# When transposed probabilities are filled and multiplied with V in an attention and mixture-of-experts kernel

## The chip, the cores and the metric

The kernel runs on one core of one Trainium2 chip. The metric is the device time of one execution in microseconds (us), lower is better. Besides plain runs there is one execution under the hardware profiler, whose records the profile and the trace show.

## The reference, cut to what matters

```python
def _attn_ref(q, k, v, f):                      # 4 batches, 8 heads, S = 576, D = 64
    scores = np.matmul(q, k.transpose(0, 1, 3, 2)) / np.sqrt(D)
    cum = np.cumsum(np.log(np.clip(f, 0.0001, 1.0)), axis=-1)
    scores = np.where(causal, -1e9, scores + cum[..., :, None] - cum[..., None, :])
    attn = np.exp(scores - np.max(scores, axis=-1, keepdims=True))
    attn = attn / (np.sum(attn, axis=-1, keepdims=True) + 1e-09)
    return np.matmul(attn, v)
```

Its output, 2304 tokens of 512 numbers, goes through a dense feed-forward layer (512 to 2048 and back, with a piecewise quadratic in between) and then through a layer of eight experts of which each token takes one. The change touches the attention and the first steps of the feed-forward part.

## The kernel before, in words

The attention works on 16 pairs of heads, and each pair on 9 tiles of 64 queries (both heads side by side, so 128 rows). There are 144 steps, n = 9 * pair + tile, and each engine has its own loop over n, written out by hand; semaphores alone join them. Every multiplication is done in three passes of a high and a low part, to keep float32 accuracy.

Tile i of a pair passes through these stages:

- PE scores it (`score`, L1304 to L1314, causal, so 64 * (i + 1) columns, and a small matmul that adds the mask) four steps ahead, n + 4. Tile 8 is too wide for one bank and has six matmuls of 288 columns (L1310).
- DVE adds the decay and takes the row minimum (`masked`, L984), three steps ahead.
- ACT takes the exponential (`exp`, L783), two steps ahead.
- PE transposes the probabilities in blocks of 128 x 128 into one of two PSUM banks (`turn`, L1329). One call is a *fill*; there are eight in a pair, numbered 0 to 7, with 2, 4, 4, 2, 4, 4, 4 and 1 transpositions, and fill k takes bank k % 2. A fill waits until DVE has emptied the bank from the fill two before (`pt_l`). Fills 0 to 7 need tiles up to 1, 3, 5, 5, 7, 7, 8 and 8.
- ACT copies a fill as the high part (`high`, L792), and DVE subtracts to get the low part (`low`, L1000), which frees the bank.
- PE multiplies with V: an early product for tiles 0 to 3 of both heads (`attend_early`), and for tiles 4 to 8 the late product a of one head and b of the other (`attend_late_a`, `attend_late_b`), all at L1345. ACT copies the early product (L798), DVE the two late ones (L1012, L1016).

Behind the last fill PE transposes the inverse denominators of the pair before (`turn_inverse`, L1337; *inverse* in short), and DVE copies them (L1006). DVE computes the denominator with its 1e-9 at tile 7 (L990) and inverts at tile 8 (L996).

Which fill runs in which step comes from the table `FILL`, whose first field is the tile that the fill needs last:

```python
FILL = ((1, 0, 1, 0, 2), (3, 0, 2, 2, 2), (5, 0, 2, 4, 2), (5, 2, 1, 4, 2),
        (7, 0, 2, 6, 2), (7, 2, 2, 6, 2), (8, 0, 4, 8, 1), (8, 4, 1, 8, 1))
```

So before, fill 0 is at tile 1, fill 1 at 3, fills 2 and 3 at 5, fills 4 and 5 at 7, fills 6 and 7 at 8, and none at tiles 0, 2, 4 and 6. The early product stands at tile 6, the late products of the pair before at tiles 2 and 4.

POOL splits q, k and v of the coming pairs into high and low parts: kh (L566), qh (L568), kl (L570), ql (L573), then v (`split_v`, L581 and L583). `split_v` waits for `late_b` of two pairs before, as it overwrites V. In eight pairs (6 to 13) one block of the attention's output is read back, multiplied on POOL with the inverse denominators (L622, L624), and split by ACT (L804) and DVE (L1021, the x split) at tile 1 of the next pair; the next such load waits for the DVE split. SP issues the loads and stores.

At the end, PE has two up blocks of the feed-forward part (12 matmuls each) at steps 142 and 143, and the DVE's first `hidden` stand at steps 146 and 148. A `hidden` is a chain of DVE hclip (L1026), ACT hpos and hsq (L829, L831), DVE g (L1029), ACT gh (L839) and DVE gl (L1031); PE needs hpos to take the up block's bank again.

## Time and profile before

| | us |
|---|---|
| runs, median of 3 (lowest to highest) | 882.01 (880.87 to 882.09) |
| the profiled execution, own time | 880.4 |
| its span | 878.4 |
| PE busy | 842.3 (96%) |
| PE weight loads busy | 796.7 (91%) |
| DVE busy | 410.5 (47%) |
| ACT busy | 394.8 (45%) |
| POOL busy | 366.4 (42%) |

The span runs from the first to the last instruction that the profiler recorded; the own time has some 2 us around it. Busy time is the union of an engine's instructions over the whole span. The attention fills about the first quarter of it, up to some 223 us, and the shares there differ from the averages in this table. Matmuls are pipelined: one starts before the one ahead of it has ended, so on PE the distance from start to start counts, not the duration.

### The profile page before, as it was taken

What the parts mean: (1) busy time and instruction counts of PE and PEld (TensorE: products, weight loads), DVE (VectorE), ACT (ScalarE), POOL (GpSimd) and SP (SyncE); (2) the same over time, 40 slices, a digit from 0 to 9 for tenths busy, and PEclk for the clock granted to TensorE, in tenths of its full rate; (3) what the DMA queues carried; (4) which work ended last, traced back from release to release, by engine and by line L of the source; (5) the groups of instructions that cost most, each with busy time, mean ns of one, the idle gap of its engine ahead of it and who ended that gap; (6) DMA issues with size and microseconds to landing.
All of it is one profiled execution on the core that took longest, in us unless ns stands there. A gap on an engine that the chain in (4) does not pass through costs nothing.

```text
span 878.4 us, 13981 instructions
## 1 busy us (share of the span) xinstructions
PE 842.3 (96%) x5138; PEld 796.7 (91%) x5139; DVE 410.5 (47%) x1001; ACT 394.8 (45%) x906; POOL 366.4 (42%) x370
## 2 busy tenths in 40 slices
PE   4999999999989999999999999999999999999995
PEld 3888888888989999999999999999998998998984
DVE  3777788886555544444444445454425210210201
ACT  4777777776566534434534444343331211211211
POOL 7755787784465411201201020074411492010394
PEclk9999999999999999999999999999999999999999
DMA  5667888872200121031021021432233364213140
GB/s 181 178 205 219 237 256 256 257 251 80 56 1 1 47 80 49 7 102 52 28 99 54 28 100 50 124 132 61 61 109 96 103 172 132 77 44 120 35 138 25
DMA packets 66334, 94.58 MB, mean 108 GB/s; under 512 B 6662, under 2 KB 42502, under 8 KB 66256
## 3 DMA queue, kind: packets, MB, share of 16 engines
q1 hardware_dynamic: 58160, 79.43, 30.0%
q10 hardware_dynamic: 6336, 9.44, 3.0%
q0 software_dynamic: 1760, 4.72, 1.4%
q8 instruction: 43, 0.70, 0.4%
q14 instruction: 35, 0.29, 0.1%
HBM read 69.82 MB, written 24.27 MB: 107 GB/s over the span
## 4 chain that ended last, share of the span: by engine, by line
PE 88%; ACT 5%; DVE 4%; issue 1%; POOL 1%; DMA 0%; SPq 0%; ACTq 0%; POOLq 0%; DVEq 0%
PE psum L1370 23%; PE psum L1372 22%; PE psum L1371 22%; PE psum L1304 6%; PE psum L1345 6%; PE psum L1329 4%; DVE ptl L1000 1%; PE psum L1310 1%; ACT pth L792 1%; ACT xo L798 1%; PE psum L1425 1%; DVE g L1029 1%; ACT pr L783 1%; PE psum L1424 1%; PE psum L1314 1%
## 5 line engine op out<-in xcount | busy, mean ns | idle before, releaser
L1370 PE MATMUL psum<-xh,winh 128*128 128x384 f32 x384 | 130.9, 341 | 3.5 <-ACT hpos L829 3.5
L1371 PE MATMUL psum<-xl,winh 128*128 128x384 f32 x384 | 128.4, 334 | 0.0
L1370 PE MATMUL psum<-gh,wouth 128*128 128x384 f32 x384 | 128.4, 334 | 0.0
L1372 PE MATMUL psum<-xh,winl 128*128 128x384 f32 x384 | 128.3, 334 | 0.0
L1372 PE MATMUL psum<-gh,woutl 128*128 128x384 f32 x384 | 128.3, 334 | 0.0
L1371 PE MATMUL psum<-gl,wouth 128*128 128x384 f32 x384 | 128.3, 334 | 0.0
L829 ACT ACTIVATE hpos<-psum,minus 128x384 f32<-128x384 f32 x96 | 55.8, 581 | 149.8 <-DVE hclip L1026 149.5
L1029 DVE TENSOR_TENSOR g<-hpos,hsq 128x384 f32<-128x384 f32 x96 | 63.3, 660 | 112.9 <-ACT hsq L831 112.9
L783 ACT ACTIVATE pr<-pr,mmin 128x64 f32<-128x64 f32 (+2 forms) x144 | 81.7, 568 | 38.3 <-DVE mmin L984 38.3
L622 POOL TENSOR_TENSOR xst<-xst 128x384 f32<-128x384 f32 x24 | 24.3, 1012 | 178.7 <-DMA xst<-rinv_d 178.7
L1142 DVE SCALAR_TENSOR_TENSOR hl<-psum,hh 128x384 fp32r<-128x384 f32 x48 | 26.7, 557 | 141.0 <-ACT hh L860 141.0
L1031 DVE TENSOR_TENSOR gl<-g,gh 128x384 fp32r<-128x384 f32 x96 | 58.4, 609 | 61.3 <-ACT gh L839 61.3
L1000 DVE TENSOR_TENSOR ptl<-psum,pth 128x512 fp32r<-128x512 f32 (+2 forms) x128 | 68.9, 570 | 35.9 <-ACT pth L792 35.3
L839 ACT CAST gh<-g 128x384 fp32r<-128x384 f32 x96 | 49.3, 514 | 75.3 <-DVE g L1029 73.8
L1370 PEld LDWEIGHTS psum<-xh,winh 128*128 128x128 f32 x384 | 72.2, 188 | 4.9 <-issue 3.5
L984 DVE CUSTOM_DVE_ANT_0 pr<-psum,c 128x64 f32<-128x64 f32 (+2 forms) x144 | 68.0, 476 | 13.4 <-PE psum L1314 13.4
L1370 PEld LDWEIGHTS psum<-gh,wouth 128*128 128x128 f32 x384 | 72.1, 188 | 0.2 <-POOL woutl L636 0.2
L1371 PEld LDWEIGHTS psum<-xl,winh 128*128 128x128 f32 x384 | 72.2, 188 | 0.0
L1329 PE MATMUL psum<-ident,pr 128*128 128x128 f32 x400 | 61.9, 281 | 10.6 <-DVE ptl L1000 10.6
L1372 PEld LDWEIGHTS psum<-xh,winl 128*128 128x128 f32 x384 | 72.1, 188 | 0.0
L1372 PEld LDWEIGHTS psum<-gh,woutl 128*128 128x128 f32 x384 | 72.1, 188 | 0.0
L1371 PEld LDWEIGHTS psum<-gl,wouth 128*128 128x128 f32 x384 | 72.1, 188 | 0.0
(216 smaller groups left out, 1938.2 us busy)
## 6 DMA issues: line engine op xcount, KB each, us to landing
praw<-moe_w SPq DMA_DIRECT2D x48, 256.0 KB, 2.7
qraw<-q SPq DMA_DIRECT2D x16, 576.0 KB, 5.5
vraw<-vk SPq DMA_DIRECT2D x16, 320.0 KB, 2.9
xh<-yh_d SPq DMA_DIRECT2D x20, 256.0 KB, 4.1
xl<-yl_d SPq DMA_DIRECT2D x20, 256.0 KB, 4.5
kraw<-k SPq DMA_DIRECT2D x16, 288.0 KB, 4.4
c<-cum_d SPq DMA_DIRECT2D x32, 144.0 KB, 4.1
xa_d<-xo SPq DMA_DIRECT2D x16, 288.0 KB, 3.7
```

The lines of the kernel that those rows point to most:

```text
L783: nc.scalar.activation(region, region, ACT.Exp, bias=mmin[:, p % 2, i:i + 1], scale=-1.0, accum_out=rsum[:, p % 2, i:i + 1]).then_inc(expe ...
L829: nc.scalar.activation(hpos[:], psum[:, UP[u % 2], 0:CH], ACT.Relu, bias=minus[:, 0:1]).then_inc(up_read, 1)
L984: nc.vector.tensor_tensor_reduce(out=out_at, in0=src, in1=c_at, scale=-SCALE, scalar=LARGE, op0=ALU.add, op1=ALU.min, accum_out=mmin[:, p ...
L1000: nc.vector.tensor_tensor(stacked(ptl, k), of_bank(k), stacked(pth, k).bitcast(F32), ALU.subtract).then_inc(pt_l, 1)
L1029: nc.vector.tensor_tensor(g[:], hpos[:], hsq[:], ALU.add).then_inc(summed, 1)
L1031: nc.vector.tensor_tensor(gl[:, u % NG, :], g[:], gh[:, u % NG, :].bitcast(F32), ALU.subtract).then_inc(g_l, 1)
L1304: nc.tensor.matmul(psum[:, bank, 0:w], q_[:, p % 2, i, :], k_[:, p % 2, 0:w], start=a == 0, stop=False)
L1329: x = nc.tensor.transpose(psum[:, PT[k % 2], at * P:(at + 1) * P], pr[:, at_tile(i) + b * P:at_tile(i) + (b + 1) * P], ident[:])
L1345: x = nc.tensor.matmul(dst[:, (i - i0) * D:ni * D], vv[:, p % 2, b, h, :], src, start=n == 0, stop=n == len(todo) - 1)
L1370: nc.tensor.matmul(psum_at, ah, bh, start=start, stop=False)
L1371: nc.tensor.matmul(psum_at, ah, bl, start=False, stop=False)
L1372: return nc.tensor.matmul(psum_at, al, bh, start=False, stop=stop)
```

## The change

A second table, `WHEN`, sets the step of each fill: tiles 1, 3, 4, 5, 6, 7, 8, and 9, which is tile 0 of the next pair. There is one fill in each step but that of tile 2. The late product b goes from tile 4 to tile 3, the early product from 6 to 5, and their copies on DVE and ACT one step earlier too. Late product a stays at tile 2. At the end, the last inverse goes from step 145 to step 146, behind late product a.

```diff
-    def fills_of(i):
-        return [k for k in range(FILLS) if FILL[k][0] == i]
+    WHEN = (1, 3, 4, 5, 6, 7, 8, 9)
+
+    def fills_at(n):
+        return [(p, k) for p in range(PAIRS) for k in range(FILLS) if NB * p + WHEN[k] == n]
+
+    def last_fill(i):
+        return max(k for k in range(FILLS) if FILL[k][0] == (i | 1 if i < 8 else 8))
...
 ACT
-            for n in range(-AHEAD, STEPS + 1):
+            for n in range(-AHEAD, STEPS + 2):
                 if 0 <= n + 2 < STEPS:
                     exp(n + 2)
-                p, i = tile_of(n - 1)
-                if 0 <= n - 1 < STEPS:
-                    for k in fills_of(i):
-                        high(p, k)
+                for p, k in fills_at(n - 1):
+                    high(p, k)
                 p, i = tile_of(n)
-                if i == 7 and 0 <= p < PAIRS:
+                if i == 6 and 0 <= p < PAIRS:
                     copy_early(p)
...
 DVE
-                p, i = tile_of(n - 1)
-                if 0 <= n - 1 < STEPS:
-                    for k in fills_of(i):
-                        low(p, k)
-                    if i == 8 and p >= 1:
+                for p, k in fills_at(n - 1):
+                    low(p, k)
+                    if k == FILLS - 1 and p >= 1:
                         copy_turned(p - 1)
...
-                if i == 5 and 0 <= p - 1 < PAIRS:
+                if i == 4 and 0 <= p - 1 < PAIRS:
                     copy_late_b(p - 1)
-                if p == PAIRS and i == 1:
+                if p == PAIRS and i == 2:
                     dve.wait_ge(turned, FILLS * PAIRS + 1)
                     copy_turned(PAIRS - 1)
...
 PE
+                for p, k in fills_at(n):
+                    turn(p, k)
                 p, i = tile_of(n)
-                if 0 <= n < STEPS:
-                    for k in fills_of(i):
-                        turn(p, k)
                 if n in UP_EARLY:
                     up_block(UP_EARLY.index(n))
-                if i == 6 and 0 <= p < PAIRS:
+                if i == 5 and 0 <= p < PAIRS:
                     attend_early(p)
                 if i == 2 and 0 <= p - 1 < PAIRS:
                     attend_late_a(p - 1)
-                if i == 4 and 0 <= p - 1 < PAIRS:
+                if i == 3 and 0 <= p - 1 < PAIRS:
                     attend_late_b(p - 1)
-                if p == PAIRS and i == 1:
+                if p == PAIRS and i == 2:
                     pe.wait_ge(pt_l, FILLS * PAIRS)
                     pe.wait_ge(r_copied, PAIRS - 1)
                     turn_inverse(PAIRS - 1).then_inc(turned, 1)
```

Three places of the order show it. The changed kernel's line numbers are two higher on PE (L1331 transposes, L1347 multiplies with V) and six higher on ACT.

PE between the score of tile 8 (288 columns) and the score of the next pair's tile 0 (64 columns), before:

```order
L1310 MATMUL psum<-kh,ql 128x288
L1314 MATMUL psum<-mask_b,ident_b 128x64
L1345 MATMUL psum<-pth,vv 128x320 x3
L1345 MATMUL psum<-pth,vv 128x192
L1345 MATMUL psum<-pth,vv 128x64
L1345 MATMUL psum<-ptl,vv 128x320 x3
L1345 MATMUL psum<-ptl,vv 128x192
L1345 MATMUL psum<-ptl,vv 128x64
L1304 MATMUL psum<-kh,qh 128x64
L1304 MATMUL psum<-kl,qh 128x64
L1304 MATMUL psum<-kh,ql 128x64
L1314 MATMUL psum<-mask_b,ident_b 128x64
```

and now, from within late product b (L1347) on:

```order
L1347 MATMUL psum<-pth,vv 128x64
L1347 MATMUL psum<-ptl,vv 128x320 x3
L1347 MATMUL psum<-ptl,vv 128x192
L1347 MATMUL psum<-ptl,vv 128x64
L1312 MATMUL psum<-kh,qh 128x288
L1312 MATMUL psum<-kl,qh 128x288
L1312 MATMUL psum<-kh,ql 128x288
L1312 MATMUL psum<-kh,qh 128x288
L1312 MATMUL psum<-kl,qh 128x288
L1312 MATMUL psum<-kh,ql 128x288
L1316 MATMUL psum<-mask_b,ident_b 128x64
L1331 MATMUL psum<-ident,pr 128x128 x4
```

Late product b stood between the two scores; now it stands ahead of the score of tile 8, and fill 2 (`128x128 x4`) behind that score.

ACT from the exponential of tile 8 (`128x576`) of a pair's end on, through the fills at the pair's last tiles, before (in this and the next fence the copies with `pth` are `high`, the one with `xo` is the early product's). The first two rows are the exponentials of tiles 7 and 8:

```order
L783 ACTIVATE pr,rsum<-pr,mmin 128x512
L783 ACTIVATE pr,rsum<-pr,mmin 128x576
L792 CAST pth<-psum 128x2x256
L792 CAST pth<-psum 128x256
L783 ACTIVATE pr,rsum<-pr,mmin 128x64
L798 COPY xo<-psum 128x2x256
L783 ACTIVATE pr,rsum<-pr,mmin 128x128
L792 CAST pth<-psum 128x2x256 x2
L783 ACTIVATE pr,rsum<-pr,mmin 128x192
L792 CAST pth<-psum 128x4x128
```

and now, with the same exponential of tile 7 first:

```order
L789 ACTIVATE pr,rsum<-pr,mmin 128x512
L798 CAST pth<-psum 128x2x256
L789 ACTIVATE pr,rsum<-pr,mmin 128x576
L798 CAST pth<-psum 128x256
L804 COPY xo<-psum 128x2x256
L789 ACTIVATE pr,rsum<-pr,mmin 128x64
L798 CAST pth<-psum 128x2x256
L789 ACTIVATE pr,rsum<-pr,mmin 128x128
L798 CAST pth<-psum 128x2x256
L789 ACTIVATE pr,rsum<-pr,mmin 128x192
L798 CAST pth<-psum 128x4x128
L789 ACTIVATE pr,rsum<-pr,mmin 128x256
```

The copy of fill 2 now stands ahead of the exponential of tile 8, that of fill 3 behind it, and no two fills' copies stand side by side.

PE at the end of the attention, from the end of the second early up block (`xh,winh`) on, before:

```order
L1370 MATMUL psum<-xh,winh 128x384
L1371 MATMUL psum<-xl,winh 128x384
L1372 MATMUL psum<-xh,winl 128x384
L1337 MATMUL psum<-ident,rinv 128x128
L1345 MATMUL psum<-pth,vv 128x320 x3
L1345 MATMUL psum<-pth,vv 128x192
L1345 MATMUL psum<-pth,vv 128x64
L1345 MATMUL psum<-ptl,vv 128x320 x3
L1345 MATMUL psum<-ptl,vv 128x192
L1345 MATMUL psum<-ptl,vv 128x64
```

and now, directly behind the same up block:

```order
L1331 MATMUL psum<-ident,pr 128x128
L1339 MATMUL psum<-ident,rinv 128x128
L1347 MATMUL psum<-pth,vv 128x320 x3
L1347 MATMUL psum<-pth,vv 128x192
L1347 MATMUL psum<-pth,vv 128x64
L1347 MATMUL psum<-ptl,vv 128x320 x3
L1347 MATMUL psum<-ptl,vv 128x192
L1347 MATMUL psum<-ptl,vv 128x64
L1339 MATMUL psum<-ident,rinv 128x128
L1347 MATMUL psum<-pth,vv 128x320 x3
```

Fill 7 of the last pair (with the inverse of the pair before it) is behind the up block, and the last inverse, which stood directly behind that block, is behind late product a.

## Rows read from the trace of the kernel before

**Rows 1.** Busy time of each engine in one pair's stretch; busy us and (x instructions).
```profile
159.70:172.40 12.70, 12.04 (x96) 10.79 (x95) 10.67 (x33) 9.79 (x28) 10.37 (x9) 1.00 0.83 254
```

**Rows 2.** Who PE waited for: us in total, times, longest us.
```profile
PE psum L1329 <- DVE ptl L1000: 10.6, 17, 0.8
```

**Rows 3.** Timeline of PE, one pair; start, duration, line, operation, count, [idle before].
```profile
159.21 0.64 PE L1329 MATMUL psum<-ident,pr 128*128 128x128 f32 x4
159.60 0.38 PE L1310 MATMUL psum<-kh,qh 128*128 128x288 f32 x1
...
160.48 0.20 PE L1314 MATMUL psum<-mask_b,ident_b 128*128 128x64 bf16 x1
160.52 0.83 PE L1345 MATMUL psum<-pth,vv 128*128 128x320 f32 x5
...
161.84 0.28 PE L1304 MATMUL psum<-kh,qh 128*128 128x64 f32 x1
...
162.83 0.31 PE L1304 MATMUL psum<-kh,qh 128*128 128x128 f32 x1
...
164.60 1.07 PE L1329 MATMUL psum<-ident,pr 128*128 128x128 f32 x8
165.43 0.36 PE L1304 MATMUL psum<-kh,qh 128*128 128x256 f32 x1
...
165.87 0.20 PE L1314 MATMUL psum<-mask_b,ident_b 128*128 128x64 bf16 x1
166.73 0.90 PE L1329 MATMUL psum<-ident,pr 128*128 128x128 f32 x5 [0.66 <-DVE ptl L1000]
167.46 0.27 PE L1337 MATMUL psum<-ident,rinv 128*128 128x128 f32 x1
...
168.66 0.20 PE L1314 MATMUL psum<-mask_b,ident_b 128*128 128x64 bf16 x1
168.85 0.41 PE L1329 MATMUL psum<-ident,pr 128*128 128x128 f32 x2
```

**Rows 4.** Timeline of ACT in the same pair.
```profile
161.90 0.78 ACT L783 ACTIVATE pr<-pr,mmin 128x576 f32<-128x576 f32 x1 [0.72 <-DVE mmin L984]
...
162.90 0.86 ACT L792 CAST pth<-psum 128x512 fp32r<-128x512 f32 x2
163.64 0.36 ACT L783 ACTIVATE pr<-pr,mmin 128x64 f32<-128x64 f32 x1
...
164.39 0.59 ACT L798 COPY xo<-psum 128x512 f32<-128x512 f32 x1 [0.30 <-PE psum L1345]
164.88 0.41 ACT L783 ACTIVATE pr<-pr,mmin 128x128 f32<-128x128 f32 x1
```

**Rows 5.** Timeline of DVE in the same pair.
```profile
164.66 0.88 DVE L990 TENSOR_SCALAR rden<-rsum 128x9 f32<-128x9 f32 x1
165.46 0.34 DVE L984 CUSTOM_DVE_ANT_0 pr<-psum,c 128x192 f32<-128x192 f32 x1
...
165.89 1.29 DVE L1000 TENSOR_TENSOR ptl<-psum,pth 128x512 fp32r<-128x512 f32 x2
...
169.42 0.73 DVE L1021 TENSOR_TENSOR xl<-xst,xh 128x384 fp32r<-128x384 f32 x1
```

**Rows 6.** Timeline of POOL in the same pair.
```profile
164.51 1.00 POOL L622 TENSOR_TENSOR xst<-xst 128x384 f32<-128x384 f32 x1
...
168.31 1.43 POOL L570 TENSOR_TENSOR kl<-kraw,kh 128x576 fp32r<-128x576 f32 x1
169.69 3.01 POOL L573 TENSOR_TENSOR ql<-qraw,qh 128x1152 fp32r<-128x1152 f32 x1
```

**Rows 7.** The denominator's line L990: durations min/median/max in ns.
```profile
L990 DVE TENSOR_SCALAR rden<-rsum x16: 168/598/882, 25.3 to 214.9; 128x9 f32<-128x9 f32 x16
```

**Rows 8.** DVE and PE at the start of the feed-forward part.
```profile
221.09 0.54 DVE L1026 TENSOR_SCALAR hclip<-psum 128x384 f32<-128x384 f32 x1
...
244.68 0.41 PE L1370 MATMUL psum<-xh,winh 128*128 128x384 f32 x1 [0.91 <-ACT hpos L829]
```

More of the change, by code:

```diff
@@ L972, in masked @@
                 if p >= 1:
-                    dve.wait_ge(turned, FILLS * (p - 1) + max(fills_of(i | 1 if i < 8 else 8)) + 1)
+                    dve.wait_ge(turned, FILLS * (p - 1) + last_fill(i) + 1)
                 if p >= 2 and i == 0:
```

## The prediction

> **What bounds the kernel now.** I read the stretches first [rows 1]. In one pair of heads, 12.70 us from one place to the same place in the next pair, TensorE (PE) is busy for 12.04 us, VectorE (DVE) for 10.67, ScalarE (ACT) for 9.79 and GpSimd (POOL) for 10.37, and the granted clock is 1.00, the full 2.4 GHz. PE sets the pace, with little idle time, and the three others have only two to three us of slack in a pair. Then the table of waits of PE [rows 2]: the transpositions (L1329) wait 17 times, 10.6 us in all, for the DVE subtraction that empties their PSUM bank. That is the prize of this change.
>
> The order of PE in time [rows 3] shows where that wait is. Fills 4 and 5 (the eight transpositions at 164.60) run side by side in step 7 and fill 6 must wait in step 8 until fill 4's bank is empty: the score of tile 3 of the next pair ends with its mask at 165.87, and PE goes on at 166.73. A mask is otherwise followed after 0.04 us (160.48 to 160.52); here the pause is 0.86, so 0.82 is lost. The listed 0.66 is less, since the end of a matmul overlaps the next one's start. Fill 7 stands directly behind fill 6: the five transpositions take 0.73 until the inverse at 167.46, where eight take 0.83 in all, 0.10 each; some 0.15 is a second wait. Fill 0 follows its mask after 0.19 (168.66 to 168.85): a third wait, of 0.15. Together **1.1 us a pair**. The pairs repeat this at a distance of 12.68 us.
>
> **What the change leaves as it is.** Every matmul, copy and subtraction stays; only places change. PE's own work even shrinks a little: four transpositions take 0.39 alone (159.21 to 159.60), so two times four 0.78, where eight side by side take 0.83; the last transposition of a fill hides under the score behind it. Fills 2 and 3, 4 and 5, 6 and 7 are parted: 3 times 0.05, **minus 0.15 a pair**.
>
> **The new queue of ACT.** What used to stand between the score of tile 8 and the score of the next pair's tile 0 was late product b, 1.32 us (160.52 to 161.84). It now stands ahead of the score of tile 8. So tile 8 is scored, and fill 2 turned, directly ahead of the next pair's tiles 0 to 3, which are PE's shortest steps. ACT holds its copy of fill 2 ahead of the exponential of tile 8, and stands idle until late product b is done. From the end of fill 2 on it has these to do in a row, by [rows 4]: copy of fill 2 (512 columns, 0.48 from start to start, the copy at 164.39 to the exponential at 164.88), the exponential of tile 8 with its accumulator 0.78 + 0.09, copy of fill 3 0.27, the early product's copy 0.48, exponential of tile 0 0.35, and the copy of fill 4, 0.59 to its end. That is 3.0 us. Ahead of it stand 0.67 (fill 2 itself, 0.39, and the end of its last matmul), behind it the DVE subtraction of 0.69 (two take 1.29 in [rows 5]) and 0.15 to PE: **4.5 us from the start of fill 2 to the start of fill 6**. PE's work in the same stretch, by [rows 3]: fill 2 0.39, score 0 0.38 (it and a fill of six, 0.61, take 0.99 from 161.84 to 162.83), fill 3 0.17 (0.39 less two times 0.11), score 1, the early product and score 2 1.77 (162.83 to 164.60), fills 4 and 5 0.78, score 3 0.48 (165.43 to 165.87 and the mask's 0.04): 3.97. **Fill 6 still waits 0.5**, against 0.82.
>
> **Fill 7 takes a new wait.** It needs fill 5's subtraction, and this stands on DVE behind the subtraction of fill 4, the denominator (L990) and the masked minimum of tile 2 (0.34, then 0.08 for its accumulator). From the start of fill 4's subtraction: 0.61 + denominator + 0.28 + 0.69 + 0.15 = 1.73 + denominator. PE gets there after 0.84 (the subtraction's rest and the hand-over) + fill 6 0.39 + score 4 0.56 = 1.79. The denominator is nine numbers wide and takes anything from 168 to 882 ns [rows 7]. The reason can be read in [rows 5, 6]: it starts at 164.66, while POOL works at 164.51 to 165.51 (L622), and ends at 165.54. It stands until POOL's instruction is over. So fill 7 waits between 0.1 and 0.8. Where the denominator meets POOL's queue in the new order isn't shown anywhere, and I take **0.35**, the middle. Fill 0 needs fill 6's subtraction: 0.67 + copy 0.62 + subtraction and hand-over 0.84 is 2.13 from fill 6's start, and ACT has an exponential (0.47 with its lead) in its way, at most 0.3 of it in series; PE is there after 0.39 + 0.56 + 0.35 + 0.17 + score 5 0.64 = 2.11. **0.0 to 0.4; I take 0.35**, since both engines' queues run without a pause here. Sum of the new waits: 0.5 + 0.35 + 0.35 = 1.2, against 1.1. With the 0.15 saved the pair would be even or shorter by 0.05; but the waits for ACT can't shrink by what PE saves (PE comes earlier and waits longer), so I charge the saving only as far as waits fall: **plus 0.1 a pair, 15 pairs: +1.5 us**. Bounds: fill 7 and fill 0 at no wait at all give 0.5 - 1.1 + (-0.15) = -0.75 a pair, -11; both full, 0.5 + 0.8 + 0.4 - 1.1 = +0.6, +9.
>
> **POOL's phase against the x split.** Eight pairs also split a chunk of x on DVE (L1021, SBUF against SBUF). At 169.42 it meets POOL's kl (168.31 to 169.74, L570), stands 0.3 for it and takes 0.73. POOL's queue is started by late product b (split_v waits for late_b), and its 3.01 us instruction ql (L573) begins at 169.69 [rows 6], 7.85 after that product ends at 161.84; the x split begins 7.58 after. Now the score of tile 8, 0.92 (159.60 to 160.52), lies between them, so the x split comes 8.5 after: inside ql, which ends at 10.86. Then DVE stands for up to 2.4 us. DVE has 2.0 us idle in a pair [rows 1], about half of it ahead of the next use, so up to **1.2 us** reaches PE. But an x split that late makes the next load of x late, POOL then adds x later and ql moves back behind the split, so it shouldn't strike every pair. Bounds 0 and 8 x 1.2 = 9.6; I take **+1.5**.
>
> The Trainium skill (SBUF — State Buffer, "SBUF: two separate sides") says that DVE and GpSimd share a port pair as an exclusive lock, held for a whole instruction, also against a DVE operation with two SBUF inputs. The denominator's end 0.03 us after POOL's agrees. By that rule the split would be held through ql each time it starts inside it; without it this term would be nil and the sum 1.5 less.
>
> **The end of the attention.** Before, fill 7 of the last pair stood ahead of the second early up block, which covered its copies, and the last inverse followed that block directly; DVE copied it and began hclip, the first step of the feed-forward chain, at 221.09 [rows 8]. Now fill 7 comes behind the up block; late product a needs its subtraction, about 1.0 us later (the transposition 0.27, a 128-column copy and a subtraction of about 0.3 each, and the hand-overs); and the inverse comes behind late product a, 1.32. The chain starts 2.3 later against PE. DVE copies the late product b one hidden earlier, which may give back 0.3. Does the shift last? PE still waits 0.91 for that chain (ACT's hpos) at 244.68 [rows 8], so yes: **+2.0**. Bounds: 0 where the chain isn't what binds, 2.4 in full.
>
> **Sum:** 1.5 + 1.5 + 2.0 = +5.0 us. The profiled execution took 880.4 us (span 878.4) and would take 885.4. The median of the runs shown is 882.0, 1.6 above it; **882.0 + 5.0 = 887.0 us**.
>
> **Rivals.**
> (a) *The lock strikes every time.* The split falls into ql in all eight pairs and the denominator into a POOL instruction in all: 9.6 + 15 x 0.2 + 2.3 is about +12 to 15, 895 us. For it: the split's new place, 0.65 us behind ql's start. Against it: the feedback through the load of x. Chance 0.2.
> (b) *The spread works: faster.* Place: the bank wait of fills 6, 7 and 0. Each fill now has two steps between itself and the one whose bank it takes. If ACT and DVE catch up in steps 0 to 3, where there's one fill less than before, fill 6 waits no more than 0.5, and 7 and 0 hardly: -0.5 a pair, -7.5, and +2.0 at the end: 876.5. It decides if the denominator is short (0.17) in most pairs and ACT's row of 3.0 us shortens by over 0.2. Against it: ACT's idle time, once PE gives it fill 2 late, can't be got back. Chance 0.12.
> (c) *Waits only change their names.* -0.1 to -0.15 a pair and +2.0 at the end: 882. Chance 0.13.
> That leaves 0.55 for the forecast, whose own range is 884 to 891.
>
> **The numbers.** About 0.2%, 1.8 us, is what can be told from no change. Faster by more: 0.12, case (b). Within it: 0.12, case (c). Slower by more: 0.76, the forecast and (a). The range that leaves out 2 in 10, the lower half of (b) and the upper half of (a), is 880.0 to 893.5.
>
> **What would show it.** The pair's distance on PE should be 12.7 to 12.9 without an x split and up to 13.6 with one; L1331 (the transpositions' new line) should wait for DVE in more places than before, at fills 6, 7 and 0, with 10 to 20 us in all. ACT should wait about 1.4 us for fill 2 in each pair. Some x splits should take over 1.5 us, ending with ql. hclip should begin about 2.3 us later behind the last up block. A distance under 12.5, or a wait of L1331 under 8 us, would refute the ACT queue; x splits of 0.7 us throughout would refute the POOL term; an unchanged distance with +2 us would leave the end alone.

## The result, and the profile after

| | before | after |
|---|---|---|
| median of 10 runs each, us | 881.58 (880.41 to 882.30) | 885.07 (883.46 to 887.42) |
| ratio of the two kernels' runs, 95% interval | | 1.0041 (1.0030 to 1.0052) |
| the profiled execution, own time, us | 880.4 | 884.11 |
| its span, us | 878.4 | 882.0 |

The change costs 3.5 us, 0.4%: slower by more than 0.2%, as forecast, and less than the forecast 5.0. The time of 885.1 us lies in the range of 880.0 to 893.5. The ten runs of the changed kernel also scatter over 4.0 us, the ten of the kernel before over 1.9; the cause isn't shown (the last section has two candidates).

The page of the changed kernel, its span and its part 1 (busy us, share of the span, instructions):

```profile
span 882.0 us, 13981 instructions
PE 843.2 (96%) x5138; PEld 798.5 (91%) x5139; DVE 416.7 (47%) x1001; ACT 392.6 (45%) x906; POOL 364.9 (41%) x370
```

The table of waits of PE, up to 300 us (in total, times, longest; us), which answers to [rows 2]:

```profile
PE psum L1331 <- DVE ptl L1004: 12.5, 40, 0.8
```

17 waits of 10.6 us have become 40 of 12.5. The spread of the fills has not shortened the wait for the bank; it has cut it in three. The timeline of PE in one pair shows the three, for comparison with [rows 3]:

```profile
89.75 0.20 PE L1316 MATMUL psum<-mask_b,ident_b 128*128 128x64 bf16 x1
90.25 0.63 PE L1331 MATMUL psum<-ident,pr 128*128 128x128 f32 x4 [0.30 <-DVE ptl L1004]
...
91.17 0.20 PE L1316 MATMUL psum<-mask_b,ident_b 128*128 128x64 bf16 x1
91.76 0.30 PE L1331 MATMUL psum<-ident,pr 128*128 128x128 f32 x1 [0.39 <-DVE ptl L1004]
91.89 0.27 PE L1339 MATMUL psum<-ident,rinv 128*128 128x128 f32 x1
...
92.53 0.20 PE L1316 MATMUL psum<-mask_b,ident_b 128*128 128x64 bf16 x1
92.93 0.41 PE L1331 MATMUL psum<-ident,pr 128*128 128x128 f32 x2 [0.20 <-DVE ptl L1004]
```

Mask to transposition, less the 0.04 that it takes without a wait: fill 6 waits 0.46, fill 7 0.55, fill 0 0.36, together 1.37 against 1.1 before. ACT and DVE in the same pair say why (answers to [rows 4, 5]):

```profile
86.47 0.59 ACT L798 CAST pth<-psum 128x512 fp32r<-128x512 f32 x1 [1.33 <-PE psum L1331]
86.95 0.78 ACT L789 ACTIVATE pr<-pr,mmin 128x576 f32<-128x576 f32 x1
...
87.72 0.36 ACT L798 CAST pth<-psum 128x256 fp32r<-128x256 f32 x1
87.98 0.59 ACT L804 COPY xo<-psum 128x512 f32<-128x512 f32 x1
88.45 0.36 ACT L789 ACTIVATE pr<-pr,mmin 128x64 f32<-128x64 f32 x1
...
88.80 0.59 ACT L798 CAST pth<-psum 128x512 fp32r<-128x512 f32 x1
```

```profile
89.42 0.69 DVE L1004 TENSOR_TENSOR ptl<-psum,pth 128x512 fp32r<-128x512 f32 x1 [0.67 <-ACT pth L798]
90.02 0.72 DVE L994 TENSOR_SCALAR rden<-rsum 128x9 f32<-128x9 f32 x1
90.66 0.34 DVE L988 CUSTOM_DVE_ANT_0 pr<-psum,c 128x192 f32<-128x192 f32 x1
...
90.93 0.68 DVE L1004 TENSOR_TENSOR ptl<-psum,pth 128x512 fp32r<-128x512 f32 x1
```

ACT stands 1.33 us for fill 2, which PE turns at 85.80, and is then busy without a pause to the copy of fill 4 (88.80, the fill turned at 88.08) and on. DVE's subtraction of fill 4 comes at 89.42 and ends at 90.11; fill 6 follows it at 90.25. Behind it stand the denominator, 0.72 for nine columns, and a masked minimum, so fill 5's subtraction starts at 90.93 and ends at 91.61, and fill 7 runs at 91.76. From the start of fill 2 to that of fill 6 it is 4.45 us, where the prediction added up 4.5.

Stretches of the changed kernel, from one place to the same place in the next pair (columns as in [rows 1]):

```profile
89.75:102.57 12.82, 11.93 (x95) 10.75 (x94) 10.06 (x32) 9.18 (x29) 7.96 (x7) 1.00 0.84 249
110.00:122.36 12.36, 11.39 (x89) 9.98 (x88) 10.54 (x35) 10.40 (x31) 9.39 (x8) 1.00 0.88 271
122.36:135.58 13.22, 12.73 (x102) 11.60 (x101) 11.14 (x32) 8.75 (x26) 11.27 (x9) 1.00 0.77 233
```

Where before every pair from the third on took 12.68, there are now three lengths: mostly 12.82 without an x split, and 12.35 or 13.22 in turn with one. The granted clock is 1.00 in all three stretches. Taken by the start of DVE's masked minimum of tile 4, the fifteen distances between the sixteen pairs compare so:

| distances | before, sum | after, sum | difference |
|---|---|---|---|
| the first (start of the attention) | 12.83 | 11.79 | -1.04 |
| six without an x split (12.82, 13.23, 12.80, 12.81, 12.82, 12.37) | 76.27 | 76.85 | +0.58 |
| eight with one (13.22, 12.35, 13.22, 12.35, 13.22, 12.35, 13.23, 13.32) | 101.43 | 103.26 | +1.83 |

The timeline of two x splits, one that passed and one that was held, and of POOL beside them (DVE, then POOL):

```profile
119.09 0.54 DVE L1025 TENSOR_TENSOR xl<-xst,xh 128x384 fp32r<-128x384 f32 x1
...
157.01 2.77 DVE L1025 TENSOR_TENSOR xl<-xst,xh 128x384 fp32r<-128x384 f32 x1
```

```profile
117.91 1.16 POOL L574 TENSOR_SCALAR qh<-qraw 128x1152 fp32r<-128x1152 f32 x1 [1.01 <-DMA qraw<-q]
119.03 1.91 POOL L576 TENSOR_TENSOR kl<-kraw,kh 128x576 fp32r<-128x576 f32 x1
120.89 2.69 POOL L579 TENSOR_TENSOR ql<-qraw,qh 128x1152 fp32r<-128x1152 f32 x1
...
155.31 1.43 POOL L576 TENSOR_TENSOR kl<-kraw,kh 128x576 fp32r<-128x576 f32 x1
156.71 2.67 POOL L579 TENSOR_TENSOR ql<-qraw,qh 128x1152 fp32r<-128x1152 f32 x1
```

Before, a split met kl and took 0.73 in seven of eight cases, 0.97 in the first [rows 5, 6]. Now five of the eight (at 105.9, 131.4, 157.0, 182.6 and 195.8) start inside ql and take 2.77 to 2.87: the one at 157.01 ends at 159.78, 0.4 after ql at 159.38. The three others take 0.54 to 0.62. After a held split the next load of x is late: SP issues it at 108.68, when the split that began at 105.88 ends (108.65), and the loads behind it in SP's queue, that of q among them (111.61), are late too. SP waits for DVE's splits (50 to 215 us; 2.0 us in 5 waits before):

```profile
SPq L423 <- DVE xl L1025: 14.4, 6, 3.3
```

So POOL waits 1.01 for qraw at 117.91, ql comes behind the next split, which passes, and the one after is held again. Only the last two are held one after the other.

What the three lengths are made of can be read on PE, from mask to mask. At a distance of 12.35 or 12.37 fill 6 still waits 0.46 (102.57 to 103.07) and fill 0 0.35, and only fill 7's wait is gone but for 0.10: 0.91 in all, some 0.2 less than before. With the 0.15 of the parted fills that makes the 0.33 that are missing from 12.68. At 12.82 the waits are 1.37, 0.27 more, less the same 0.15. A held split adds 0.96 to the 12.35, in the steps behind it: the mask of tile 1 follows that of tile 0 after 2.11 instead of 1.51, in which fill 3 waits 0.39 for fill 1's subtraction, which comes late (111.30 to 111.99; the fill is at 112.14), and the two steps up to tiles 3 and 4 take 0.12 and 0.24 more. The denominator is 0.16 there and spares 0.10: 13.21.

The end of the attention, PE and DVE (answers to [rows 8]):

```profile
222.22 0.27 PE L1331 MATMUL psum<-ident,pr 128*128 128x128 f32 x1
222.33 0.27 PE L1339 MATMUL psum<-ident,rinv 128*128 128x128 f32 x1
223.28 0.85 PE L1347 MATMUL psum<-pth,vv 128*128 128x320 f32 x5 [0.68 <-DVE ptl L1004]
...
224.63 0.33 PE L1339 MATMUL psum<-ident,rinv 128*128 128x128 f32 x1
```

```profile
225.20 0.54 DVE L1030 TENSOR_SCALAR hclip<-psum 128x384 f32<-128x384 f32 x1
```

hclip starts at 225.20 instead of 221.09, 4.1 later. The next four vary between 3.3 and 4.5, and from the sixth hidden on all are 3.7 late, which is the difference of the two spans but for 0.1. So the whole loss arises in the attention and in the first steps behind it. One thing differs beside the order. In the changed kernel's trace the granted clock is at half (1.2 GHz) for 3.4 us, from 231.8 on, with PE busy for 1.39 us of the 2 from 230 to 232; the trace of before has no such dip. It cost nothing there: the hclips of the changed kernel are 3.3 to 3.4 us behind those of e3 (below) on both sides of it. In e3's own trace the dip comes at some 265, with PE busy throughout, and costs 1.5. So spans of single traces can differ by 1.5 us that is not of the order; the first hclip lies ahead of the dip in every trace here. Of the 25 runs of the kernel before beside e1 to e4, the six with a mean clock of 0.999 take 880.4 to 881.0, as the profiled one does, and those with 0.995 to 0.997 take 880.9 to 883.7.

### The profile page after: what moved, and what is told of

Same layout as the page of the kernel before. It is cut to its first block, busy times and chain, and to the rows that moved or that the text cites. A ratio compares the mean times of both kernels' runs of the same rounds, so it can differ in the third digit from the quotient of the medians.

```text
span 882.0 us, 13981 instructions
## 1 busy us (share of the span) xinstructions
PE 843.2 (96%) x5138; PEld 798.5 (91%) x5139; DVE 416.7 (47%) x1001; ACT 392.6 (45%) x906; POOL 364.9 (41%) x370
## 4 chain that ended last, share of the span: by engine, by line
PE 79%; ACT 9%; DVE 6%; issue 4%; POOL 1%; DMA 0%; SPq 0%; DVEq 0%; ACTq 0%; POOLq 0%
PE psum L1372 23%; PE psum L1373 22%; PE psum L1374 22%; PE psum L1347 4%; PE psum L1306 3%; ACT pth L798 3%; ACT pr L789 3%; PE psum L1331 2%; DVE ptl L1004 2%; PE psum L1312 1%; ACT xo L804 1%; DVE g L1033 1%; DVE pr L988 1%; PE psum L1426 1%; PE psum L1425 1%
## 5 line engine op out<-in xcount | busy, mean ns | idle before, releaser
L1004 DVE TENSOR_TENSOR ptl<-psum,pth 128x512 fp32r<-128x512 f32 (+2 forms) x128 | 73.2, 572 | 30.0 <-ACT pth L798 28.1
L1331 PE MATMUL psum<-ident,pr 128*128 128x128 f32 x400 | 68.6, 283 | 13.1 <-DVE ptl L1004 12.5
L798 ACT CAST pth<-psum 128x512 fp32r<-128x512 f32 (+2 forms) x128 | 61.7, 482 | 24.1 <-PE psum L1331 22.4
```

The costliest lines, as they stand in the source:

```text
L798: nc.scalar.copy(stacked(pth, k), of_bank(k)).then_inc(pt_h, 1)
L1004: nc.vector.tensor_tensor(stacked(ptl, k), of_bank(k), stacked(pth, k).bitcast(F32), ALU.subtract).then_inc(pt_l, 1)
L1331: x = nc.tensor.transpose(psum[:, PT[k % 2], at * P:(at + 1) * P], pr[:, at_tile(i) + b * P:at_tile(i) + (b + 1) * P], ident[:])
```

## The experiments

All medians stand beside runs of the kernel before on the same chip (881.55 for e1 to e4, 882.16 for e5 to e7 and c1, 881.56 for e8, e9, c3 and the second c1); ratios are to it, and are estimated from all single runs, so that they can differ a little from those of the medians. Line numbers in the diffs' kernels are those of the changed kernel, unless said otherwise.

### The two halves of the change

**e1, the fills alone.** The changed kernel with both products back at their places of before:

```diff
 ACT  -                if i == 6 and 0 <= p < PAIRS:   +  if i == 7   (copy_early)
 DVE  -                if i == 4 and 0 <= p - 1 < PAIRS:   +  if i == 5   (copy_late_b)
 PE   -                if i == 5 and 0 <= p < PAIRS:   +  if i == 6   (attend_early)
 PE   -                if i == 3 and 0 <= p - 1 < PAIRS:   +  if i == 4   (attend_late_b)
```

> The changed kernel with the early product back at tile 6 and late product b back at tile 4 (copies too): only the fills are spread. Theory Q (the queues of ACT and DVE decide, and the place of late product b ahead of the score of tile 8 is what makes ACT stand and then run without a pause): the waits of fill 7 and fill 0 shrink, the pair's distance is 12.6 to 12.7 us (12.68 before, 12.82 and 12.36/13.21 in the changed kernel), and with the end of the attention as in the change the time is 1 to 3 us above before. Rival S (the spread of the fills itself costs, wherever the products stand): distance 12.8 as in the change, +3.5 us or more.

Measured: 884.37 us, ratio 1.0026 (1.0017 to 1.0036), +2.3 us by the ratio and +2.8 by the medians. The table of waits of PE between 50 and 300 us:

```profile
PE psum L1331 <- ACT pr L789: 8.4, 13, 1.3
...
PE psum L1331 <- DVE ptl L1004: 0.6, 2, 0.4
```

It looks as if a wait for the exponential had taken the place of the wait for the bank, but the table names only who signalled last. In one pair, PE, ACT and DVE:

```profile
87.11 0.63 PE L1331 MATMUL psum<-ident,pr 128*128 128x128 f32 x4 [0.59 <-ACT pr L789]
```

```profile
85.66 0.59 ACT L798 CAST pth<-psum 128x512 fp32r<-128x512 f32 x1 [1.30 <-PE psum L1347]
```

```profile
86.28 0.69 DVE L1004 TENSOR_TENSOR ptl<-psum,pth 128x512 fp32r<-128x512 f32 x1 [1.24 <-ACT pth L798]
```

Fill 4 at 87.11, 0.74 late behind its mask at 86.33, needs the exponential of tile 7, and that had ended at 84.27. The one that ends, with its accumulator, at 87.01 is tile 8's, which it doesn't need. What it does need is the bank of fill 2, whose subtraction ends at 86.97, 0.14 ahead of it. ACT had made fill 2's copy wait 1.30 for late product b, since the copy overwrites what that product reads. So it is still the bank, now in front of fill 4; fill 6 doesn't wait, fills 7 and 0 wait 0.30 and 0.24. That is 1.28 in all, 0.18 more than before, and the 0.15 of the parted fills comes off it: the fourteen distances behind the first come to 0.4 us more than before (12.67 in the eight pairs with an x split, 12.70 to 12.74 in most others). In the pairs, that is rival (c). hclip is 2.2 later in this trace. The first distance is 1.5 shorter, and from the last pair's masked minimum to hclip, the end of the attention, it takes 3.4 longer. From the sixth hidden on the delay is 4.1, and how much of that is the clock's dip (at 244 here) isn't parted.

**e2, the products alone.** The kernel before with the early product at tile 5 and late product b at tile 3, copies one step earlier, fills untouched:

```diff
 ACT  -                if i == 7 and 0 <= p < PAIRS:   +  if i == 6   (copy_early)
 DVE  -                if i == 5 and 0 <= p - 1 < PAIRS:   +  if i == 4   (copy_late_b)
 PE   -                if i == 6 and 0 <= p < PAIRS:   +  if i == 5   (attend_early)
 PE   -                if i == 4 and 0 <= p - 1 < PAIRS:   +  if i == 3   (attend_late_b)
```

> The kernel before with only the products moved (early at tile 5, late b at tile 3, copies one step earlier), fills as before. Theory Q: fills 2 and 3 stand behind the score of tile 8, which is now behind late product b; so ACT gets six transposed blocks at once, late, ahead of the exponential of tile 8, and the row of work up to fill 4 and fill 6 grows: the distance goes from 12.68 to 13.7 to 14.2, the time up by 12 to 19 us. Rival S (only the fills' spread costs): within 1 us of before.

Measured: 893.93 us (4 runs), ratio 1.0141 (1.0124 to 1.0158), +12.4 us. The timeline of PE with the transpositions of one pair, then the stretch of a pair (columns as in [rows 1]):

```profile
78.15 1.06 PE L1329 MATMUL psum<-ident,pr 128*128 128x128 f32 x8 [0.28 <-DVE ptl L1000]
79.41 0.20 PE L1314 MATMUL psum<-mask_b,ident_b 128*128 128x64 bf16 x1
...
80.89 0.90 PE L1329 MATMUL psum<-ident,pr 128*128 128x128 f32 x5 [1.27 <-DVE ptl L1000]
```

```profile
76.84:90.58 13.74, 12.18 (x95) 10.86 (x95) 10.48 (x31) 9.27 (x28) 8.00 (x7) 1.00 0.60 192
```

Fill 6 now waits from 79.45 to 80.89, 1.44, and fills 4 and 5 wait too. ACT stood 1.66 us for the masked minimum of tile 8 (at 75.94), since late product b delays that tile's score, and it enters the steps of tiles 0 to 3 with that much more to do. The fourteen distances behind the first are 13.6 on average (13.25 to 14.27), a little under the 13.7 to 14.2 that were expected. So the two parts don't add up: alone they cost +2.3 and +12.4, together +3.5. The products' new place is what makes ACT late, as the prediction's third step said, and the spread of the fills pays back most of it. In this order too some x splits are held in ql (1.6 to 2.66 us in seven of eight), and what that costs here was not parted.

### The end of the attention

**e3.** The changed kernel with fill 7 of the last pair and the last inverse back one step:

```diff
-        return [(p, k) for p in range(PAIRS) for k in range(FILLS) if NB * p + WHEN[k] == n]
+        return [(p, k) for p in range(PAIRS) for k in range(FILLS) if NB * p + WHEN[k] - (p == PAIRS - 1 and k == FILLS - 1) == n]
 DVE, PE
-                if p == PAIRS and i == 2:
+                if p == PAIRS and i == 1:
```

> The changed kernel, with the last pair's fill 7 again in step 143 ahead of the second early up block, and the last inverse again in step 145 directly behind it. Theory Q: the pairs keep their distances of 12.82 and 12.36/13.21, hclip starts 1.7 us after that of before instead of 4.1, and the time falls by 1.7 to 2.2 us against the changed kernel, to 1.5 to 2 above before. Rival (the feed-forward chain absorbs the end anyway): no change against the changed kernel, +3.5.

Measured: 882.39 us, ratio 1.0009 (0.9997 to 1.0021), 2.7 us less than the changed kernel, where 1.7 to 2.2 were expected; it can't be told from before. DVE:

```profile
221.63 0.28 DVE L1010 COPY rturn<-psum 9x128 f32<-9x128 f32 x1 [0.75 <-PE psum L1339]
221.83 0.54 DVE L1030 TENSOR_SCALAR hclip<-psum 128x384 f32<-128x384 f32 x1
```

hclip starts 3.37 us earlier than in the changed kernel, and 0.74 after that of before instead of the expected 1.7. Of the 3.37, 1.14 is already there at the masked minimum of the last pair's tile 4, nearly all because the eighth x split (at 195.75) took 0.54 in this execution and not 2.87; **2.2 us belong to the end itself**. The other distances are the same to within 0.05.

### The denominator

**e4.** The changed kernel without the denominator: the inverse is taken of the row sum itself. It leaves out the addition of 1e-9.

```diff
-                    act.wait_ge(den_ok, p - 1)
+                    act.wait_ge(inv_ok, p - 1)
...
-                dve.wait_ge(den_ok, p + 1)
+                dve.wait_ge(exped, NB * (p + 1))
...
-                nc.vector.reciprocal(rinv[:, p % 2, 0:NB], rden[:, p % 2, :]).then_inc(inv_ok, 1)
+                nc.vector.reciprocal(rinv[:, p % 2, 0:NB], rsum[:, p % 2, :]).then_inc(inv_ok, 1)
...
-                if i == 7 and 0 <= p < PAIRS:
-                    denominator(p)
```

> The changed kernel without L994: DVE takes the reciprocal of the row sums directly. It leaves out the addition of 1e-9 to the row sums. Theory Q: in the pairs without an x split, fill 7's second wait (0.6 us, behind a denominator of 0.72) disappears, the distance falls from 12.82 to 12.3; the pairs with an x split have a denominator of 0.16 to 0.28 already and change by less than 0.3 each. Time 2.5 to 4.5 us below the changed kernel, about as before. Rival (the denominator is hidden, fill 7 waits for ACT): distance stays 12.82, time less than 0.5 lower.

Measured: 879.98 us, ratio 0.9982 (0.9971 to 0.9993), 5.1 us less than the changed kernel, a little more than expected. The wait of L1329, the transpositions' line here, up to 300 us, fell from 12.5 us in 40 to:

```profile
PE psum L1329 <- DVE ptl L1004: 9.9, 34, 0.5
```

The pairs take 12.25 instead of 12.82 without an x split: fill 7 no longer waits. Of the 5.35 us up to the last pair's masked minimum, 3.4 come from the six distances without a split, and these are the denominator's. 0.8 come from the first; there PE's matmuls keep the slow pace of the start (0.38 from one of 448 columns to the next, 0.20 later) up to some 20.0 in the changed kernel's trace and 18.1 in this one. And 1.1 come from the eight with a split, where four were held and not five.

**e5.** The same edit in the kernel before (again without the addition of 1e-9).

> The kernel before without L990, the reciprocal taken of the row sums directly; it leaves out the addition of 1e-9. Theory Q: in the kernel before, fill 6 waits for the pure latency of fill 4's copy and subtraction, and the denominator is hidden (two pairs had it at 168 ns and the same distance), so the distance stays 12.68 and the time within 1 us of before. Rival (the denominator costs the same in any order): distance falls by 0.3 to 0.5, time by 4 to 6 us.

Measured: 881.58 us, ratio 0.9995 (0.9986 to 1.0005), and every distance still 12.68. In the old order the same instruction, up to 0.88 long [rows 7], costs nothing. The likely reason is that fill 7 follows fill 6 directly and both have waited by then. So what the distances without a split gained in e4 is the price of the denominator's place between the subtractions of fills 4 and 5, not of the instruction.

### The x split and POOL's ql

**e6.** e4 with the x split, on ACT and DVE, at tile 0 instead of 1.

```diff
 ACT, DVE
-                if p - 1 in X_LOADED and i == 1:
+                if p - 1 in X_LOADED and i == 0:
```

> e4 (the changed kernel without the 1e-9 addition, which is left out) with ACT's and DVE's halves of the x split at tile 0 instead of tile 1. In e4 the split took 2.75 to 2.89 us in four of eight pairs, held through POOL's ql, and distances of 13.2 to 13.3 stood beside 12.25. Theory P (the port decides): at tile 0 the split meets kl or qh, takes at most 1.4, the long distances of 13.3 disappear or shrink below 12.9, and the time falls by 1 to 4 us against e4. Rival (the split's own work and place cost, not POOL): 13.3 stays in half of the pairs or more, time as in e4 or above.

Measured: 880.73 us, ratio 0.9982 (0.9973 to 0.9992), no different from e4. The splits no longer fall into ql, and the distances of 13.3 are gone, as expected; but the time isn't, which was a miss. DVE and PE:

```profile
113.19 0.69 DVE L1004 TENSOR_TENSOR ptl<-psum,pth 128x512 fp32r<-128x512 f32 x1
113.79 1.05 DVE L1025 TENSOR_TENSOR xl<-xst,xh 128x384 fp32r<-128x384 f32 x1
...
115.18 0.28 DVE L1004 TENSOR_TENSOR ptl<-psum,pth 128x128 fp32r<-128x128 f32 x1
```

```profile
115.51 0.70 PE L1345 MATMUL psum<-pth,vv 128*128 128x320 f32 x3 [0.42 <-DVE ptl L1004]
```

Each split meets kl, takes 1.05 and stands between the subtractions of fills 6 and 7; late product a, which needs fill 7's, waits for it. Seven distances are 12.85, the one with the first split is 13.21 and the one behind the last 11.88. Over these nine that is 0.7 more than in e4, where four are 13.19 to 13.33 and five 12.24 or 12.25.

**e8.** e4 with ql in two instructions, of four and five tiles of queries:

```diff
-                nc.gpsimd.tensor_tensor(ql[:, par], qraw[:], qh[:, par].bitcast(F32), ALU.subtract).then_inc(q_l, 1)
+                nc.gpsimd.tensor_tensor(ql[:, par, 0:4], qraw[:, 0:4], qh[:, par, 0:4].bitcast(F32), ALU.subtract)
+                nc.gpsimd.tensor_tensor(ql[:, par, 4:NB], qraw[:, 4:NB], qh[:, par, 4:NB].bitcast(F32),
+                                        ALU.subtract).then_inc(q_l, 1)
```

> e4 (the changed kernel without the 1e-9 addition, which is left out), with POOL's ql as two instructions of four and five query tiles, so that the port comes free in between. Theory P: the x splits that took 2.75 to 2.89 us take at most 1.9, the distances of 13.3 fall to 12.3 to 12.8, and the time is 1 to 4 us below e4's (880.0). Rival (a split blocked in ql costs only DVE idle time, or POOL's own chain sets 13.3): 13.3 stays in half of the pairs, time within 1 us of e4.

Measured: 875.84 us (4 runs), ratio 0.9931 (0.9916 to 0.9946), 4.1 us less than e4. POOL and DVE (lines two higher from there on):

```profile
102.58 1.31 POOL L579 TENSOR_TENSOR ql<-qraw,qh 128x512 fp32r<-128x512 f32 x1
103.83 1.91 POOL L580 TENSOR_TENSOR ql<-qraw,qh 128x640 fp32r<-128x640 f32 x1
```

```profile
102.79 1.52 DVE L1027 TENSOR_TENSOR xl<-xst,xh 128x384 fp32r<-128x384 f32 x1
```

The split still starts inside ql, but now ends 0.42 after the first half's end at 103.89; DVE has the 1.5 us to spare, and all fourteen distances behind the first are 12.24. The second half of ql takes 1.91 where its median over all pairs is 1.57. The fourteen distances are 4.2 us shorter than e4's, which is the long instruction's price by itself: four held splits in e4, about 1.05 each. Whether ql in two gains as much with the denominator in its place was not tried, nor whether it gains anything in the kernel before, where no split was held in ql.

### Both costs together, and a better order

**e9** is e3 and e4 in one (no addition of 1e-9).

> e3 and e4 together (the addition of 1e-9 is left out): do the two costs add? If the end (2.7 us) and the denominator (5.1 us) are separate, 877 to 878, about 4.5 below before. Rival (both are paid in the feed-forward chain's slack): 879.5 or more.

Measured: 877.37 us (4 runs), ratio 0.9949 (0.9932 to 0.9966). It lies 2.6 us under e4 and 5.0 under e3, as expected (the two ran on other chips, whose runs of before agree to 0.1 us), so the end and the denominator's place are separate costs.

**c1** and **e7** try another order: fills at tiles 2, 4, 4, 5, 6, 7, 8, 8, the early product at 7, the late ones at 3 and 4, the end as before. c1 is without the denominator's addition of 1e-9, e7 with it.

```diff
-    WHEN = (1, 3, 4, 5, 6, 7, 8, 9)
+    WHEN = (2, 4, 4, 5, 6, 7, 8, 8)
```

> A version meant to beat both: fills at tiles 2, 4, 4, 5, 6, 7, 8, 8, early product at 7, late product a at 3 and b at 4 (copies one step later each), the end as in the kernel before, no denominator (the addition of 1e-9 is left out). Late product b stays behind the score of tile 8, but the fills are spread, so that fill 6 has two steps to fill 4. Theory Q: fill 6's wait goes (0.86 to 0), waits of 0.7 us remain at fills 3 to 5, distance 12.2 to 12.3, 5 to 7 us below before. Rival S (spreading as such costs): 12.7 or more, no gain.

> The candidate's order with the denominator as in the kernel before. Theory Q with the port: fill 7's subtraction stands behind the denominator again, which takes 0.7 in pairs without an x split: distance 12.2 to 12.4 in the eight pairs with one, 12.7 to 13.0 in the others, time 0 to 4 us below before, 2 to 5 above the candidate. Rival (the denominator is hidden in this order too): as the candidate, within 1 us.

Measured: c1 875.33 us (4 runs), ratio 0.9922 (0.9906 to 0.9939), distance 12.29; e7 880.42 us, ratio 0.9980 (0.9971 to 0.9990), distance 12.95 where the denominator takes 0.78 and 12.35 in the last eight, where it takes 0.16 (13.33 with one of 1.16, and 12.81 with one of 0.17, which stands apart). It is the same price as in e4, in another order of the fills. The split never falls into ql in these two. A second measurement of c1 beside the last candidate gave 876.46 us and 0.9937 (0.9924 to 0.9951): half a microsecond over the expected time, within the expected ratio, and not over the 877 that would have put the first result down to its chip.

> The first candidate once more, in five rounds (the addition of 1e-9 is left out): 875 to 876, ratio 0.991 to 0.994, distance 12.29. If the first result was one chip's, over 877.

**c3** keeps a fill in most steps, but starts later: fills at tiles 2, 4, 5, 5, 6, 7, 8, 9, late products at 3 and 4, the early one at 5, the end as in e3, and no addition of 1e-9. Of the diff only the order of fills and late products on PE is shown; the late products' copies go one step later too.

```diff
-    WHEN = (1, 3, 4, 5, 6, 7, 8, 9)
+    WHEN = (2, 4, 5, 5, 6, 7, 8, 9)
...
 PE
-                if i == 2 and 0 <= p - 1 < PAIRS:
-                    attend_late_a(p - 1)
                 if i == 3 and 0 <= p - 1 < PAIRS:
+                    attend_late_a(p - 1)
+                if i == 4 and 0 <= p - 1 < PAIRS:
                     attend_late_b(p - 1)
```

> A second candidate (the addition of 1e-9 is left out): fills at tiles 2, 4, 5, 5, 6, 7, 8, 9, early product at 5, late a at 3, late b at 4, the end as before. By the queues, the first candidate's waits for tile 7's exponential (6.8 us in 15) shrink, since the early product's copy leaves ACT's row ahead of fill 4: distance 12.1 to 12.3, time 873.5 to 876.5. Rival: the x split falls into ql in some pairs and those take 13, time 878 or more.

Measured: 874.09 us (4 runs), ratio 0.9920 (0.9904 to 0.9935), 0.8% under the kernel before and the lowest median here; c1 on the same chip took 876.46, with an interval that overlaps. The waits of the transpositions for DVE between 50 and 300 us, and the stretch of a pair:

```profile
PE psum L1329 <- DVE ptl L1004: 3.6, 14, 0.3
```

```profile
80.00:92.07 12.07, 11.77 (x94) 10.70 (x94) 9.24 (x31) 9.46 (x27) 8.09 (x6) 1.00 0.71 209
```

PE is busy for 11.77 of 12.07 us, where it was 12.04 of 12.70 before [rows 1]. With another 0.3 us in one wait the transpositions wait 3.9 us in all; in c1 they wait 7.2, of which the table puts 5.6 down to an exponential. As in e1 that is the wrong name: fill 4 at 97.40 starts 0.15 after fill 2's subtraction ends (97.25), and tile 7's exponential was long over. Not every pair takes 12.07: the fourteen distances behind the first lie between 11.97 and 12.61, but for one of 13.00. No split is held in ql, so the 13.00 isn't the rival's; its cause stays open. Which of its edits brought how much was not parted. All kernels here that beat the one before leave out the addition of 1e-9, but for e7 (0.9980).

## Why the prediction was right, and where it was off

The direction, the size of some 0.5% and the places of the costs held; the sum was 1.5 us too high. Two of the three terms came near with part of their working wrong, and that is luck. By its steps:

- **The wait today** (1.1 us a pair) and **PE's own work** stand, as both orders' rows show.
- **The new queue of ACT** (fill 6 would still wait 0.5): measured 0.46. ACT stands 1.33 for fill 2 where 1.4 was said, and e2 shows the cause by itself: with the products moved and nothing else, the kernel loses 12.4 us.
- **Fill 7's new wait**, taken at 0.35 between 0.1 and 0.8: 0.55 in pairs without an x split, with a denominator of 0.72, 0.10 where the denominator takes 0.28 and none where it takes 0.16. e4, e5 and e7 confirm that it is the denominator, and in this place only. What wasn't foreseen is that the denominator is short in the pairs with an x split (and in the one ahead of them). There it meets POOL's kh near its end (0.28), or POOL between two instructions or idle (0.16). The held splits aren't the reason, since e1 and e7 hold none in ql and have 0.16 in all these pairs.
- **Fill 0's wait**, 0.35: measured 0.36.
- **Sum of the pair's waits**: +0.1 forecast, +0.58 over the six distances without a split, 0.10 each. The number agrees by two misses. The waits came to 1.37 and not 1.2, and the 0.15 that PE saves counted in full, where the prediction argued that it couldn't. Over the six, one pair is 13.23 long, with a denominator of 1.13, and one at 12.37 goes the other way.
- **The x split**, the term that carried most doubt. It does fall into ql, is held to ql's end, and the late load does push ql back, so that it doesn't strike each time: five of eight. The eight distances are 1.83 longer than before; forecast were 0.8 + 1.5 = 2.3. Held distances (13.22 to 13.32) stay under the 13.6 that was named as their limit. But the 1.5 is not what the holding costs: a held split costs about 0.9 to 1.07 (13.22 against 12.35 here, 13.32 against 12.25 in e4), so five cost some 4.5, three times the term. Against it stand pairs that are 0.33 shorter than before where the split isn't held, which the prediction had at no place. Together they leave the 1.83.
- **The end**: +2.0 forecast, with 2.3 as the shift of hclip behind PE. hclip starts 2.98 behind the start of the first instruction after the last up block, against 0.52 before, 2.5 more; e3 puts the end at 2.2 in the traces and 2.7 in the medians. Of the shift 3.7 of 4.1 lasts.
- **The start**: nothing was forecast. The first distance is 1.04 shorter, 11.79 against 12.83. Some of it is only that the masked minimum of tile 4 now comes ahead of other work; from the last pair's masked minimum to hclip e3 takes 0.6 us longer than before (at 0.14 later there, 0.74 at hclip). So about 0.5 is a real gain. PE's waits for the bank between the masks of tiles 2 and 6 of the second pair agree: 1.61 before (fills 4, 6 and 0: 0.39, 0.96, 0.26), 1.10 now. **This is the missing term.** It isn't the slow pace of PE's first matmuls, which ends at some 19.4 before and 20.0 now. Either half of the change shortens this distance (11.36 in e1, 12.07 in e2); why was not tested.

Added up at hclip: 0.58 + 1.83 for the distances, 2.2 for the end (2.83 from the last pair's masked minimum on, less e3's 0.6), and -0.5 for the start make 4.1; the forecast's 1.5 + 1.5 + 2.0 = 5.0. Behind hclip 0.4 is given back, which leaves the 3.7 that the spans show.

One of the prediction's own signs spoke against it: a distance under 12.5 would refute the ACT queue, and five of the fourteen are 12.35 or 12.37. The queue is still there, as fill 6 waits 0.46 in such a pair too; the sign was set too high, since it left out a short denominator. (The case of no change also has a chance of 0.13 in one place and 0.12 in the other.)

Of the rivals, (a), the lock at every split, asked for eight of eight and +12; five of eight came, and +3.5. Rival (c), waits that only move, happened for the fills without the products (e1). Rival (b) named its own condition, a short denominator: where it is short and the split isn't held, the pair takes 12.35, 0.33 less than before. e8, which removes the denominator and halves the holding instruction, has 12.24 in all pairs but the first and, with the changed kernel's slow end still in it, takes 875.84 us, close to the 876.5 worked out for (b). So the new order, fills and products together, is worth some 0.4 us a pair, and VectorE's collisions with GpSimd and the end take it away. The fills alone aren't worth that: e1 has 12.67 with a denominator of 0.16 and no split held in ql.

## What to carry over

A short instruction may be free where everything behind it has to wait anyway, and cost its full length where a buffer's release is behind it: before spreading work over steps, list what stands on the releasing engine between two releases, and how long each of these can be held by another engine. Where two engines hold each other up for a whole instruction, try to cut the longer instruction in two; here that gained 4.1 us (in a kernel without the denominator) where moving the shorter one gained nothing. The table of waits names who signalled last, not who was needed; compare it with what the code waits for. A software pipeline that is moved by a step needs its last round looked at by itself; here that round was at least 2.2 of 3.5 us.

## What was unexpected of the hardware

- A DVE instruction of nine columns (L994, fp32, SBUF to SBUF, one input) takes anything from 160 to 1128 ns, and its end follows that of POOL's instruction: at 90.02 it runs for 0.72 to 90.74, while POOL's kl (1.43 from 89.29) ends at 90.72. In both kernels all 24 that take 0.2 us or more end 0.02 to 0.04 us after the end of the POOL instruction in which they start. The reciprocal of the same nine columns (L1000) takes 0.20 at 91.54, in the midst of ql. The trace's row for the first, all 16:

```profile
L994 DVE TENSOR_SCALAR rden<-rsum x16: 160/276/1128, 26.1 to 218.2; 128x9 f32<-128x9 f32 x16
```

- The Trainium skill (SBUF — State Buffer, "SBUF: two separate sides") names as what takes the shared port a DVE operation with two SBUF inputs or one in a two-port mode. By that rule the two operations that were held here would be those; the x split has two SBUF inputs, and agrees. Which mode the denominator ran in no run here shows.
- Whether a split is held turns on some hundredths of a microsecond. It passed when it started 0.06 behind kl (119.09 to 119.03) and, in e3, 0.10 behind ql (195.75 to 195.65), which then took 3.19 instead of 2.69; in e4 it passed at 0.17 behind ql (165.99), which took 3.25, and was held at 0.19 behind (101.66). In every trace here a split that was held by a POOL instruction ended 0.40 to 0.43 after it. One held split more or less is about 1 us, which may be why the changed kernel's runs scatter over 4.0 us and those of before over 1.9. The dip of the clock, which costs between nothing and 1.5 us by where it falls, is the other candidate; 25 runs of the kernel before on one chip scatter over 3.3. Neither was tested run by run.
- A held split makes itself rare: the load behind it is late, POOL's next chain waits 1.0 us for qraw, and the next split passes ahead of ql. The result is a period of two pairs, 13.22 and 12.35, that no single pair's timeline shows.
